# Decayed keys and normalised rows turned by VectorE in 32 by 32 blocks and carried through memory, in place of TensorE transposes

## The reference, cut to what matters

```
f = sigmoid(f_logit)
for t in range(768):
    state = f[t][:, None] * state + outer(k[t], v[t])
    y[t] = q[t] @ state
x  = y as rows [3072, 384];  xn = x / rms(x) * rms_g
g  = xn @ w_gate                       # 384 -> 1536
x2 = (g * sigmoid(g) * (xn @ w_val)) @ w_out
h  = x2 @ w_in                         # 384 -> 2048
out = clamp_square(h) @ w_out2
```

## Time and profile before

| | |
|---|---|
| median of 3 runs | 977.84 us |
| the profiled execution, its own time | 976.92 us |
| its span, first to last instruction | 975.2 us |
| PE busy | 959.0 us (98%) |
| DVE busy | 573.8 us (59%) |
| ACT busy | 326.1 us (33%) |
| PE in the chain that ended last | 94% |
| granted TensorE clock | 1.00 |
| first tile of the first MLP | about 37 to 110 us |
| tiles 2 to 7 | 69.2 us each, to about 521 us |
| tile 8, with no attention woven in | to about 582 us |

### The profile page before, as it was taken

The page is one execution under the profiler, slowest core; times in us unless marked ns, Lnnn a source line. Parts: engine busy times, 40 slices in busy tenths (PEclk is TensorE's granted clock), DMA queues, the critical chain, the costliest instruction groups (busy, mean ns, idle before and its releaser), DMA issues.

```text
span 975.2 us, 19135 instructions
## 1 busy us (share of the span) xinstructions
PE 959.0 (98%) x7651; PEld 868.6 (89%) x7651; DVE 573.8 (59%) x1098; ACT 326.1 (33%) x556; POOL 22.5 (2%) x58
## 2 busy tenths in 40 slices
PE   6899999999999999999999999999999999999998
PEld 5899999999999999999999998888888888888886
DVE  8788666565674765765664665545545455445443
ACT  2433322322322322223223453333333343333333
POOL 0100000000000000000000000000000000000000
PEclk9999999999999999999999999999999999999999
DMA  5541111011111120210111310000000000000000
GB/s 195 181 161 43 41 42 50 32 48 40 40 40 40 40 73 8 72 41 21 60 40 49 122 57 1 1 33 0 0 32 0 0 32 0 32 0 0 32 1 33
DMA packets 16766, 42.32 MB, mean 43 GB/s; under 512 B 1376, under 2 KB 7648, under 8 KB 16736
## 3 DMA queue, kind: packets, MB, share of 16 engines
q1 hardware_dynamic: 16736, 41.88, 12.6%
HBM read 37.16 MB, written 4.72 MB: 43 GB/s over the span
## 4 chain that ended last, share of the span: by engine, by line
PE 94%; DVE 3%; issue 1%; POOL 0%; ACT 0%; DMA 0%; DVEq 0%; POOLq 0%
PE gate_ps L416 15%; PE val_ps L416 15%; PE acc L492 13%; PE gate_ps L480 10%; PE val_ps L480 10%; PE acc L438 10%; PE acc L496 7%; PE acc L442 5%; PE tb L327 2%; PE y_ps L351 2%; PE y_ps L357 2%; PE tb L337 1%; DVE qd L738 1%; PE ta L313 1%; DVE after L717 1%
## 5 line engine op out<-in xcount | busy, mean ns | idle before, releaser
L658 ACT ACTIVATE raw<-raw,half_col 128x512 f32<-128x512 f32 x96 | 69.4, 722 | 155.3 <-DVE raw L909 155.3
L492 PE MATMUL acc<-high,low 128*128 128x512 f32 x285 | 110.9, 389 | 0.0
L492 PE MATMUL acc<-high 128*128 128x512 f32 x285 | 110.9, 389 | 0.0
L597 ACT ACTIVATE act_buf<-gate_ps 128x384 f32<-128x384 f32 x96 | 47.2, 492 | 177.1 <-PE gate_ps L416 177.1
L602 ACT ACTIVATE high<-h_buf 128x384 fp32r<-128x384 f32 x96 | 50.5, 526 | 167.2 <-DVE h_buf L849 167.2
L416 PE MATMUL gate_ps<-high 128*128 (+1 forms) x288 | 99.3, 345 | 1.0 <-issue 0.6
L438 PE MATMUL acc<-high 128*128 128x384 f32 x288 | 99.1, 344 | 0.0
L416 PE MATMUL val_ps<-high 128*128 (+1 forms) x288 | 99.1, 344 | 0.0
L416 PE MATMUL gate_ps<-high,low 128*128 (+1 forms) x288 | 96.5, 335 | 0.0
L416 PE MATMUL val_ps<-high,low 128*128 (+1 forms) x288 | 96.4, 335 | 0.0
L416 PE MATMUL gate_ps<-low,high 128*128 (+1 forms) x288 | 96.4, 335 | 0.0
(11 more groups left out here) (119 smaller groups left out, 1906.8 us busy)
## 6 DMA issues: line engine op xcount, KB each, us to landing
raw<-qkf_dram SPq DMA_DIRECT2D x21, 768.0 KB, 4.3
x_all<-wb_dram SPq DMA_DIRECT2D x12, 576.0 KB, 5.0
v_sb<-v_dram SPq DMA_DIRECT2D x24, 192.0 KB, 2.8
out_dram<-x_all SPq DMA_DIRECT2D x5, 768.0 KB, 3.8
raw<-wc_dram SPq DMA_DIRECT2D x7, 384.0 KB, 3.1
x_all<-qkf_dram SPq DMA_DIRECT2D x2, 768.0 KB, 6.5
kd<-wc_dram SPq DMA_DIRECT2D x3, 384.0 KB, 2.9
qd<-wc_dram SPq DMA_DIRECT2D x3, 384.0 KB, 3.6
```

The costliest lines, as they stand in the source:

```text
L492: pe.matmul(acc[:, m, 0:N2], wc_part(w, j, 1, m), h2_hi[:, j % 2, :], start=(j == 0 and w is w_hi), stop=False)
L658: nc.scalar.activation(act2_buf[:, j % 2, :], act2_buf[:, j % 2, :], ACT.Square, bias=half_col[:, :], scale=0.5).then_inc(square_ready, 1)
```

## The change

For the chunks from 3 on (those woven into tiles), both transposes leave TensorE. VectorE transposes kd inside 32 by 32 blocks (`block_kd`, o 3, one instruction on 128x512, ahead of `decay_q`) and the normalised rows likewise (`block_x`, o 11, one on 128x384, straight behind `normalise`, which moves from o 12 to o 11). SP then stores the blocks to a buffer off the chip, waits for that to land, and issues four loads that bring the blocks back, each to 32 partitions (`move_kd`, `move_x`). ScalarE no longer copies kdT; `round_x` and `rest_x` read the loaded xT in place of PSUM and move from o 14 to o 15; `square_sum` moves from o 11 to 10, `decay_state` from o 5 to 6. `update` issues 16 matmuls of 32 or 16 output columns in place of 8 of 48, for all chunks. Buffers are shared: the kd blocks lie in `after`, the x blocks in `decayed`, xT in `scores`. In the last part of SP's program the loads of the second MLP's weights come behind the last `move_x`.

```diff
+        kd_blocks = after_words[:, 0:NB, 0:C]
-        kdT = sb("kdT", [P, NP, PR])
+        kdT = sb("kdT", [P, NB, NP, BS])
+        xT = scores[:, 0, 0:KM, :].rearrange("f k t -> f (k t)").rearrange("f (a k t) -> f a k t", a=NB, k=KM)
+        x_blocks = decayed[:, :, :].rearrange("p a e -> p (a e)")
...
+                def move_kd(n):
+                    sp.wait_ge(kd_blocks_ready, n - (CT - 1))
+                    sp.wait_ge(update_made, n)
+                    sp.dma_start(kd_dram, kd_blocks).then_inc(kd_stored, 16)
+                    sp.wait_ge(kd_stored, (n - (CT - 1)) * 16)
+                    for b in range(NB):
+                        sp.dma_start(kdT[b * BS:(b + 1) * BS, :, :, :].rearrange("t a p d -> t a (p d)"),
+                                     kd_dram.rearrange("(a t) b m -> b t a m", a=NB)[b]).then_inc(kdT_loaded, 16)
+
+                def move_x(n):
+                    sp.wait_ge(x_blocks_ready, n - (CT - 1))
+                    sp.wait_ge(x_lo_ready, n)
+                    sp.dma_start(x_dram.rearrange("t b m -> t (b m)"), x_blocks).then_inc(x_stored, 16)
+                    sp.wait_ge(x_stored, (n - (CT - 1)) * 16)
+                    for b in range(NB):
+                        sp.dma_start(xT[b * BS:(b + 1) * BS].rearrange("f a k t -> f a (k t)"),
+                                     x_dram.rearrange("(a t) b m -> b t a m", a=NB)[b]).then_inc(xT_loaded, 16)
...
                 load_wb(8)
+                move_kd(CT)
                 sp.wait_ge(qd_ready, CT + 1)
                 load_raw(CT + 1)
                 load_wb(9)
...
                 load_wb(11)
-                with sp.Fori(CT + 2, NCH) as n:
-                    sp.wait_ge(qd_ready, n)
-                    load_raw(n)
-                    sp.wait_ge(y_made, n * 2)
-                    load_v(n)
+                move_x(CT)
+                with sp.Fori(CT + 1, NCH - 1) as n:
+                    move_kd(n)
+                    sp.wait_ge(qd_ready, n + 1)
+                    load_raw(n + 1)
+                    sp.wait_ge(y_made, n * 2 + 2)
+                    load_v(n + 1)
+                    move_x(n)
...
                     for p in range(NP):
-                        for r in range(2):
-                            mm = pe.matmul(tb[r * HP:r * HP + D, p * D:(p + 1) * D], kdT[:, p, r * HP:r * HP + D],
-                                           v_sb[:, r, p, :], start=True, stop=True)
+                        for a in range(NB):
+                            m = min(BS, a // 2 * HP + D - a * BS)
+                            mm = pe.matmul(tb[a * BS:a * BS + m, p * D:(p + 1) * D], kdT[:, a, p, 0:m],
+                                           v_sb[:, a // 2, p, :], start=True, stop=True)
...
-                        if o == 4:
-                            turn_kd(n, c)
-                        elif o == 6:
+                        if o == 6:
                             score(n, c)
...
-                        elif o == 13:
-                            turn_x(n)
...
+                def block_kd(n, c):
+                    dve.wait_ge(kd_ready, n + 1)
+                    dve.wait_ge(whole_made, n + 1)
+                    nc.vector.transpose(kd_blocks.rearrange("d b (p t) -> d p b t", p=NP),
+                                        kd[:, c % 2, :, :].rearrange("d p (b t) -> d p b t", b=NB))\
+                        .then_inc(kd_blocks_ready, 1)
+
+                def block_x(n):
+                    dve.wait_ge(xs_ready, n + 1)
+                    nc.vector.transpose(x_blocks.rearrange("t (b k f) -> t k b f", b=NB, k=KM),
+                                        xs[:, :].rearrange("t (k b f) -> t k b f", k=KM, b=NB))\
+                        .then_inc(x_blocks_ready, 1)
```

More of the change, by code:

```diff
@@ L48 @@
 NW = JB * WB
+BS = 32
+NB = P // BS
+MOVED = 16 * NB
 NX = NW
@@ L106, in build @@
         xs = sb("xs", [P, DM])
[L107 to L113, removed]
+        xT = scores[:, 0, 0:KM, :].rearrange("f k t -> f (k t)").rearrange("f (a k t) -> f a k t", a=NB, k=KM)
+        x_blocks = decayed[:, :, :].rearrange("p a e -> p (a e)")
+        columns = sb("columns", [P, 7])
+        ssq, mean, rstd, minus_half, eps_col, half_col, unused = (columns[:, k:k + 1] for k in range(7))
         g_rows = sb("g_rows", [P, DM])
@@ L320, in score @@
                         pe.wait_ge(state_ready, n)
-                    if not first:
+                    if not first and isinstance(n, int) and n == CT:
                         pe.wait_ge(x_lo_ready, n)
-                    pe.wait_ge(kdT_ready, n + 1)
+                    if first:
+                        pe.wait_ge(kdT_ready, n + 1)
+                    else:
+                        pe.wait_ge(kd_ready, n + 1)
+                        pe.wait_ge(state_ready, n)
                     for p in range(NP):
@@ L714, in decay_after @@
                         dve.wait_ge(kd_ready, n)
+                    if not isinstance(n, int) or n > CT:
+                        dve.wait_ge(kd_stored, (n - CT) * 16)
                     for p in range(NP):
@@ L758, in decay_state @@
                         dve.wait_ge(y_made, n * 2)
+                    if not isinstance(n, int) or n > CT:
+                        dve.wait_ge(x_stored, (n - CT) * 16)
                     if c > 0:
@@ L768, in mask_scores @@
                     dve.wait_ge(scores_made, n + 1)
+                    if not isinstance(n, int) or n > CT:
+                        dve.wait_ge(x_lo_ready, n)
                     nc.vector.tensor_tensor(scores[:, r, :, :],
@@ L805, in rest_x @@
                     at = (slice(None), i % 2, slice(None), slice(c * C, (c + 1) * C))
-                    nc.vector.tensor_tensor(x_lo[at], bank[:, 0:KM * P].rearrange("p (k t) -> p k t", k=KM),
-                                            x_hi[at].bitcast(F32), ALU.subtract).then_inc(x_lo_ready, 1)
+                    if bank is None:
+                        rows = xT.rearrange("f a k t -> f k a t")
+                        x_lo_at, x_hi_at = (x[at].rearrange("f k (a t) -> f k a t", a=NB) for x in (x_lo, x_hi))
+                    else:
+                        rows = bank[:, 0:KM * P].rearrange("p (k t) -> p k t", k=KM)
+                        x_lo_at, x_hi_at = x_lo[at], x_hi[at]
+                    nc.vector.tensor_tensor(x_lo_at, rows, x_hi_at.bitcast(F32), ALU.subtract)\
+                        .then_inc(x_lo_ready, 1)
                 def attention(i, slot):
@@ L818, in attention @@
                         elif o == 3:
+                            block_kd(n, c)
                             decay_q(n, c)
-                        elif o == 5:
+                        elif o == 6:
                             decay_state(i, c)
@@ L826, in attention @@
                             update_state(n)
-                        elif o == 12:
+                        elif o == 11:
                             normalise(n)
-                        elif o == 14:
+                            block_x(n)
+                        elif o == 15:
                             rest_x(i, c)
```

62 lines of the change are left out of this document (43 added, 19 removed).

## The result

| | before | after |
|---|---|---|
| median of 4 runs | 977.87 us (976.65 to 978.01) | 1004.86 us (1004.33 to 1008.02) |
| the profiled execution, its span | 976.92, 975.2 | 1004.33, 1002.8 |
| first tile ends (`copy_x2` reads `acc`) | 109.68 | 122.78 |
| the next six tiles, mean | 69.15 us | 71.56 us |
| from the last of them to the end of the span | 450.6 | 450.7 |

After over before is 1.0292, 95% interval 1.0279 to 1.0304: 27 us slower, where 31 were forecast. The spans of the two profiled executions stand 27.6 us apart, and that divides cleanly: 13.1 in the first tile, 14.4 in the next six, nothing behind them. Of all the executions behind this document two, one of the kernel before and one of the kernel with all three mends, ran at a granted clock of 0.59 and 0.56 and took over 1500 us; the ratios leave them out.

The account below looks back on a forecast made before the run. PE was taken to set the pace, busy all 69.20 us of a tile. Six steady tiles +18.3, first tile +12.95 and first three chunks +0.2 gave +31.4 on 976.92: 1008.3, as a median 1009 us; range 991 to 1026.

Parts of the forecast that it names:

- Rivals 1 and 5: 1: VectorE's work and trips covered, 966 us, chance 0.07; 5: effects cancel to within 0.2%, chance 0.03.
- Rival 2: Dear VectorE transposes, at the upper bound or the skill's proportion: 20 us more in seven tiles, 1029 us; chance 0.15.
- Rival 3: Cheap steady tiles, with transposes at half price and short load issues: 1.45 us a tile, 998 us; chance 0.2.
- rival 4: The first tile's queue costs nothing, the store overtaking the weights: 9.5 us less, 1000 us; chance 0.1.
- The price of a transpose: On VectorE, 0.60 us for block_kd and 0.48 for block_x, taken from elementwise instructions of the same sizes.
- A: Block 1 of a steady tile: L442 waits for rest_h, now behind block_kd, +0.6 us.
- B: Blocks 3 to 5 of a steady tile: use_gate of block 4 comes later and PE's gate waits, +1.1 us.
- C: Blocks 6 to 8 of a steady tile: normalise waits ahead of the scans, use_gate of block 7 later, +0.9 us.
- The updates: In each chunk's update, 32 records over groups of 32 take 0.05 us less than now; -0.15 us a tile.
- D: End of a steady tile: the next tile's gate waits for chunk 2's rows to return through rest_x, +0.6 us.
- A steady tile: The four places where VectorE's new work meets PE, less the updates' gain: +3.05 us a tile, +18.3 for six.
- The first tile: SP's queue delays keys (+2.8) and rows (+6.7) behind weight loads, with 1.1 and 2.35 more: +12.95 us.

Follow-up runs that it names:

- all three mends: The changed kernel with both first-tile moves ahead of the weight loads, block_kd and decay_q at o 5, rows of chunks 0 and 1 at o 12: 984.4 us.
- the first experiment: The changed kernel with the first tile's two moves put ahead of weight loads 8 and 11 in SP's program: 997.63 us, ratio 1.0216.
- half of the edit, placed with care: The changed kernel with only keys carried, block_kd and decay_q at o 5, first-tile move ahead of weight load 8, rows on TensorE: 968.0 us, ratio 0.9905.
- the first control: The changed kernel with all transposes back on TensorE, keeping only the new form of update and 128-wide key transposes: 987.1 us, ratio 1.0093.
- the two controls: The changed kernel with all transposes back on TensorE and the new update kept: 987.1 us; the same with decay_q moved from o 3 to o 5: 984.2 us.

## Why the prediction was right, and where its terms were off

The direction, the mechanism and the places held; the sum was 31.4 against 27.4 in the profiled executions. Rivals 1 and 5 fell with the first comparison. Rival 2 fell with the transposes' 0.70 and 0.58 us. Rival 3 fell with them too, since they cost what I took and not half, though its short issues of the loads came nearer than mine; rival 4 fell with the 8.1 us of the queue. By its own steps:

- **The price of a transpose.** Taken as the elementwise one, 0.60 and 0.48 from start to start; measured 0.61 to 0.63 and 0.50 to 0.51. The Trainium skill ("VectorE: DVE Perf Modes", The three transpose paths), taken in proportion from its bf16 figure, would have been an estimate of 1.24 and 0.93. The runs decide against that use of it for float32 in blocks of 32.
- **A, +0.6.** L442 of block 1, now L483, began 5.94 us into the tile and begins 6.39 into it (343.67 less 337.28): +0.45. DVE reached the place 0.12 sooner than before (341.88, 4.60 into the tile, against 321.94, 4.72).
- **B, +1.1.** The gate's second matmul stood 25.04 us into the tile and stands 26.66 into it: 1.62 in all, less A's 0.45 is +1.17. The first update is in that span; without its gain B is +1.31.
- **C, +0.9.** 42.92 has become 45.52: 2.60 in all, so +0.98, and then 0.40 comes back with `turn_kd` of chunk 2, which leaves +0.58, or +0.72 without the update in it. The mechanism is the one forecast, `normalise` waiting ahead of the scans.
- **The updates, -0.15 a tile.** From first start of `update` to first start of `attend` is 0.35 us (351.95 to 352.30) where it was 0.49 (331.45 to 331.94): -0.14 a chunk and -0.42 a tile, three times my term. I had read sixteen of the new form from start to last end; it is the distance to the next group that counts.
- **D, +0.6.** What is left of the tile's 2.4 for it is +0.2 with the third update in it, +0.34 without. With the updates it is the term furthest off. The wait for `rest_x` is the one forecast; its size was not. From `normalise` (396.90) to the end of `rest_x` (404.80) are 7.9 us where I had 8.7: a load's issue takes 0.44 us (four in 1.76), not 0.6, so the last goes out 1.3 us behind the first, not 1.8, and store and loads land in 1.9 us each, not 2.1 and 2.2. On the other side the gate starts 0.4 behind `rest_x`, which I had put at nothing. That the issues were an estimate from a plainer kind was said; I took the dear end without a row for it. The rule of the Trainium skill on what a transfer costs ("DMA: Bandwidth & Descriptors", Anatomy of one DMA), by which D would have been dearer still, is not borne out by the rows' transfers: they land sooner by some 0.2 to 0.5 us. Nor did the landings of rows 11 agree with it within 0.4 us, as I wrote: by the rule the load of 576 KB takes 3.4 us and the store of 256 KB 2.6, and they took 5.0 and 2.1. The page of the kernel after, its DMA issues (KB each, median us to landing):

```profile
x_turn_dram<-decayed SPq DMA_DIRECT2D x21, 192.0 KB, 1.9
scores<-x_turn_dram SPq DMA_DIRECT2D x84, 48.0 KB, 1.9
```

- **A steady tile, +3.05.** With the updates apart, 0.45 + 1.31 + 0.72 + 0.34 - 0.42 is 2.4, the mean of the six measured: 14.4, not 18.3. That difference of 3.9 us is nearly the whole miss; the updates and D make up 0.27 and 0.26 of the 0.65 us in each tile, A and C 0.15 and 0.18, and B gives 0.21 back.
- **The first tile, +12.95.** Measured +13.1, but that the two agree so well is partly luck. The keys' wait is 2.80 as forecast. For the rows 9.6 us were forecast from the issue of weight block 11 to L442, and 9.54 came (70.70 to 80.24). PE, however, reached that place 5.4 us behind the issue and not 3.5, so its wait was 4.18 and not 6.1; the granted clock fell to 0.50 and took some 2.5 us more behind it, which I had not thought of and which filled the gap up to the 6.7 of the sum. That the order in the queue is the cause, the first experiment shows: with the moves ahead of the weights both waits are gone, and with them 8.1 of the 13.1.

Of the signs named ahead some were off: tiles of 72 us were said and 71.5 came; the wait at `project_out` of block 4 was to be 6 or more and was 4.18; and the wait of the next tile's gate for `rest_x` is there, but small. I had also named 1.5 us for the waits at the gates of blocks 5 and 8; they are 0.87 and 1.17, the rest of B standing at the L483 just ahead, in a row of its own (0.67).

Not tried: rows carried without DVE's work in stretch B. They share buffers (`x_blocks` with `decayed`, xT with `scores`), so a later place needs more memory first.

## What to carry to other kernels

Work taken from the bounding engine pays only if the engine that gets it is not the next to be waited for at that place: with the same instructions, other offsets were worth 1.1 and 0.6 us a tile here, and half of the edit, placed with care, made the kernel 1% faster where the whole made it 3% slower. Price moved work stretch by stretch between the two engines' timelines, not by busy shares. And look at each queue that a new transfer enters: behind large loads that nobody needed so soon, two small moves cost 8 us of a 13 us loss.

## What the runs showed of the hardware, unexpected

**The clock after a wait.** The windows of the kernel after, behind the 4.18 us wait:

```profile
80.00:82.00 2.00, 1.76 (x5) 1.58 (x6) 1.97 (x5) 0.81 (x2) 0.00 (x0) 0.50 0.23 68
82.00:84.00 2.00, 2.00 (x8) 2.00 (x8) 2.00 (x3) 0.27 (x1) 0.00 (x0) 0.50 0.65 134
84.00:86.00 2.00, 2.00 (x9) 2.00 (x8) 0.64 (x2) 1.48 (x2) 0.00 (x0) 0.60 0.82 323
86.00:90.00 4.00, 4.00 (x141) 3.68 (x140) 2.75 (x5) 1.54 (x5) 0.81 (x1) 1.00 0.02 4
```

The granted clock is 0.50, the 1.2 GHz level of the two, from 80 to beyond 84 us, while PE works without a gap. Its timeline shows the steps between large matmuls, 0.32 us here and 0.17 again at the end:

```profile
82.05 0.52 PE L457 MATMUL gate_ps<-high,low 128*128 128x384 f32 x1
82.37 0.52 PE L457 MATMUL gate_ps<-high 128*128 128x384 f32 x1
...
85.94 0.34 PE L457 MATMUL val_ps<-high 128*128 128x384 f32 x1
86.12 0.33 PE L457 MATMUL val_ps<-low,high 128*128 128x384 f32 x1
```

From 80.24 to 85.57 sixteen of them start, which would take 2.8 us at 0.17 each, so the wait of 4.18 us cost about 2.5 more. The length of a wait alone does not tell what follows: the same level came behind the wait of only 1.95 us in the first control, but behind those of 2.80 and 2.29 us in this kernel's first tile the clock stayed at 1.00, as it did behind the waits of up to 1.17 us in the steady tile above.

**Instruction packets and a wait at a loop's branch.** The 1.4 to 1.95 us in each pass behind a branch back, in the two controls, with 69 packets for 23, came with no change in what PE computes there. The Trainium skill ("Runtime: NRT & Kernel Launch", Instruction fetch mechanics) says that a taken branch to a target outside the part held forces a fetch; the place of these waits agrees, but no run here shows which loops are hit.

**Two tiny costs.** A transpose of 128x32 costs VectorE 0.20 us and one of 128x512, sixteen times as much, 0.70, so there is a fixed part of some 0.16 (an estimate from these two). And an `update` of 32 matmul records over groups of 32 columns holds PE for 0.35 us where 16 over groups of 48 held it for 0.49; sixteen more records of the first kind added 0.26.
